# One step of side work per tile, and the second half's convolution inside the first pass, in a two-layer mixture-of-experts kernel

## What is computed

```python
# attention-like convolution: x (2, 3584, 192), 8 heads of 24 channels, 7 taps per token and head
w = softmax(weight_gen)                       # (2, 3584, 8, 7)
out[b, s, h, :] = sum_k w[b, s, h, k] * x_pad[b, s + k, h, :]
# first mixture of experts: 7168 tokens, 8 experts, 192 -> 1024 -> 192, the two best of noisy logits
noisy = x @ w_gate + log1p(exp(x @ w_noise)) * noise
out[t] = sum over the 2 best e of  share_e * (relu(x[t] @ w1[e]) @ w2[e])
# second mixture of experts: the same sizes, the one best expert, times its softmax value
```

## Time and profile before

| | |
|---|---|
| runs | 1349.66, 1350.25, 1351.6 us; median 1350.25 |
| the profiled execution | 1347.76 us, its span 1346.0 us, mean granted clock 0.926 |
| busy: PE, DVE, ACT, POOL | 1165.7, 789.3, 508.5, 507.8 us |
| front, until PE's first expert matmul | 0 to 206.8 us |
| pass 0, pass 1, pass 2, pass 3 | from 206.8, 553.8, 916.8, 1146.8 us |

### The profile page before, as it was taken

The page is one execution under the profiler, slowest core; times in us unless marked ns, Lnnn a source line. Parts: engine busy times, 40 slices in busy tenths (PEclk is TensorE's granted clock), DMA queues, the critical chain, the costliest instruction groups (busy, mean ns, idle before and its releaser), DMA issues.

```text
span 1346.0 us, 25668 instructions
## 1 busy us (share of the span) xinstructions
PE 1165.7 (87%) x8376; PEld 1109.0 (82%) x8377; DVE 789.3 (59%) x1628; ACT 508.5 (38%) x997; POOL 507.8 (38%) x624
## 2 busy tenths in 40 slices
PE   3844799998779999999999988799899859899996
PEld 2531468998779999999999978799899859899996
DVE  9979984655664554544453565554553685455542
ACT  2240125432323444444454233244554324445432
POOL 1000003443334455444433444344433444455543
PEclk9975898998899999999999989899999979999988
DMA  7230133322213333262321243234631383343321
GB/s 221 63 131 4 51 109 100 92 63 75 87 32 95 97 102 99 83 245 83 95 85 53 83 137 107 72 100 150 225 93 61 92 228 91 106 141 106 104 76 31
DMA packets 96257, 136.83 MB, mean 102 GB/s; under 512 B 25930, under 2 KB 75917, under 8 KB 95948
## 3 DMA queue, kind: packets, MB, share of 16 engines
q1 hardware_dynamic: 76652, 92.96, 22.8%
q0 software_dynamic: 19552, 43.30, 10.8%
HBM read 105.00 MB, written 34.54 MB: 104 GB/s over the span
## 4 chain that ended last, share of the span: by engine, by line
PE 67%; DVE 21%; issue 5%; ACT 2%; DMA 2%; DVEq 1%; POOL 1%; SPq 0%; ACTq 0%; POOLq 0%; PEldq 0%
PE ps_y L1211 23%; PE ps_y L1212 10%; DVE prod L525 6%; PE ps_h L1189 6%; PE ps_h L1190 5%; PE ps_h L1193 5%; PE ps_h L1199 5%; PE ps_h L1196 5%; DVE prod L537 3%; PE ps_x L1175 2%; PE ps_x L1176 2%; DVE x_pad L670 2%; DVE x_pad L669 1%; DVE w_hl L737 1%; PE ps_route L1125 1%
## 5 line engine op out<-in xcount | busy, mean ns | idle before, releaser
L1211 PE MATMUL ps_y<-w_hl,h_hi 128*128 128x384 f32 x1480 | 470.5, 380 | 78.2 <-DVE h_lo L752 78.0
L1212 PE MATMUL ps_y<-w_hl,h_lo 128*128 128x192 f32 x1480 | 381.5, 258 | 0.0
L752 DVE SCALAR_TENSOR_TENSOR h_lo<-ps_h,h_hi 128x512 fp32r<-128x512 f32 (+1 forms) x404 | 240.6, 639 | 225.8 <-ACT h_hi L993 217.2
L1211 PEld LDWEIGHTS ps_y<-w_hl,h_hi 128*128 128x128 f32 x1480 | 292.8, 198 | 82.9 <-DVE h_lo L752 82.9
L993 ACT ACTIVATE h_hi<-ps_h 128x512 fp32r<-128x512 f32 (+1 forms) x404 | 204.8, 559 | 310.7 <-PE ps_h L1199 310.7
L1212 PEld LDWEIGHTS ps_y<-w_hl,h_lo 128*128 128x128 f32 x1480 | 297.1, 201 | 0.0
L436 POOL DMA_INDIRECT row<-x_rows,read_now x204 | 209.0, 1025 | 123.2 <-POOL read_now L432 84.2
L1189 PE MATMUL ps_h<-xa_hi,w1a_hi 128*128 128x256 f32 (+1 forms) x808 | 234.4, 290 | 5.1 <-issue 3.7
L1190 PE MATMUL ps_h<-xa_hi,w1a_lo 128*128 128x256 f32 (+1 forms) x808 | 231.4, 286 | 0.0
L1193 PE MATMUL ps_h<-xa_lo,w1a_hi 128*128 128x256 f32 (+1 forms) x808 | 231.0, 286 | 0.0
L1196 PE MATMUL ps_h<-xb_hh,w1b_hl 128*128 128x256 f32 (+1 forms) x808 | 230.7, 285 | 0.0
(11 more groups left out here) (168 smaller groups left out, 1411.2 us busy)
## 6 DMA issues: line engine op xcount, KB each, us to landing
w_raw<-in_moe_w_dram SPq DMA_DIRECT2D x32, 768.0 KB, 6.9
w1a_raw<-in_moe_w_dram SPq DMA_DIRECT2D x32, 512.0 KB
w1b_raw<-in_moe_w_dram SPq DMA_DIRECT2D x64, 256.0 KB, 3.9
x_pad<-in_x_dram SPq DMA_DIRECT2D x2, 2688.0 KB, 10.0
x_rows<-tok SPq DMA_DIRECT2D x14, 384.0 KB, 2.7
x_pad<-y_rows SPq DMA_DIRECT2D x8, 672.0 KB, 11.7
prod<-y_rows SPq DMA_DIRECT2D x8, 672.0 KB, 13.4
x_rows<-tok SPq DMA_DIRECT2D x4, 1344.0 KB, 8.7
```

The source lines that it names most:

```text
L752: nc.vector.scalar_tensor_tensor(out=h_lo[:, i * GF:(i + 1) * GF, 0:rows], in0=ps_h[:, i, :].rearrange("p (f t) -> p f t", f=GF)[:, :, 0:r ...
L1211: nc.tensor.matmul(ps_y[:, u, 0:2 * D], h_hi[:, i, cols], w2_hl[b][:, f, :], start=(i == 0), stop=False)
L1212: last = nc.tensor.matmul(ps_y[:, u, 0:D], h_lo[:, i, cols], w2_hl[b][:, f, 0:D], start=False, stop=(i == FC - 1))
```

## The change

- `convolution(1, ...)` and PE's `front(1, ...)` leave the front. In pass 0, tiles 0 to 13, DVE makes two columns a tile (`conv_column`): one multiply of 1344 elements (7 taps by 192 channels, read from `x_pad` with the tap as the fastest index) and one reduction over the taps. The first half of it (column 0) stands in `side_a`, ahead of the tile's `h_lo`, the second in `side_b`, ahead of the tile's `y`.
- The results of passes 1 and 2's previous half are weighted (ACT) and combined (DVE) four columns a tile. In all three passes ACT copies the tile's columns to a staging place (`stage_columns`), PE transposes them in the next tile (`turn_columns`, after the first 10 of the tile's hidden matmuls), ACT reads them (`read_turned`, between the second and third `h_hi`), and PE makes their logits in the tile after (`score_columns`). The transposes share PSUM with those of the next rows, which therefore wait for a new semaphore `ps_x_free`.
- `place` is cut in three, and the marks are made 14 to a tile (`mark_some`: 7 in `side_a`, 7 in `side_b`), with `find_some` on PE a tile later.
- `load_y` and the stores of `x_rows` (but for half 0's first) move from SP to ACT: `load_y` in tile 0 of passes 1 and 2, the stores at the end of tile 15 of pass 0, in tile 15 of pass 1 and in tile 14 of pass 2.
- ACT and DVE always handle 256 rows, also in a half-full tile; PE still does 128 there. In pass 2 the last tile no longer transposes rows for pass 3: pass 3 begins with it.
- The first expert's weights are split on DVE ahead of `place(0)` (two parts) and behind `list_rows(0)` (the third) instead of within `convolution(1, ...)`.

The table and the main functions:

```diff
+        AHEAD = 4
...
+        COLS = (2, AHEAD, AHEAD)
+        FIRST = (0, 3, 2)
+        LAST = tuple(FIRST[p] + TP // COLS[p] - 1 for p in range(PASSES - 1))
+        SCORE = tuple(LAST[p] + 2 for p in range(PASSES - 1))
+        COUNT = (SCORE[0] + 3, SCORE[1] + 1, SCORE[2] + 1)
+        MARK = (COUNT[0] + 2, COUNT[1] + 3, COUNT[2] + 3)
+        MARKS = 7
+        MARK_STEPS = tuple(TP * choices_of // (2 * MARKS) for choices_of in (2, 1, 1))
+        LIST = tuple(MARK[p] + MARK_STEPS[p] for p in range(PASSES - 1))
...
+            def conv_column(j, i):
+                dve.wait_ge(x_loaded, 96)
+                t = first_column(0, j, 0) + i
+                made = prod[:, i * K * D:(i + 1) * K * D].rearrange("p (d k) -> p d k", k=K)
+                nc.vector.tensor_tensor(
+                    made.rearrange("p (h g) k -> p h g k", g=G),
+                    x_pad[:, bass.ds(t * D, K * D)].rearrange("p (k h g) -> p h g k", h=H, g=G),
+                    taps[1][:, bass.ds(t * H, H), :].unsqueeze(2).broadcast_to([P, H, G, K]),
+                    ALU.mult).then_inc(columns_made, 1)
+                dve.wait_ge(columns_made, j * 2 + (i + 1))
+                nc.vector.tensor_reduce(tok[1][:, bass.ds(t, 1), :].rearrange("p o d -> p (o d)"), made, AX, ALU.add)\
+                    .then_inc(columns_done[1], 1)
...
+            def load_y(p, g0):
+                c = p - 1
+                act.wait_ge(y_scattered, (g0 + 1) * SUBS16)
+                act.wait_ge(found_ready, p + 1)
+                for g in range(GROUPS):
+                    for k in range(2):
...
+                        nc.scalar.dma_start(results[k][:, g * TG:(g + 1) * TG, :], src[:, g * TG:(g + 1) * TG, :])\
+                            .then_inc(y_loaded[c], 16)
+            def weight(p, j):
...
+                act.wait_ge(y_loaded[c], 2 * GROUPS * 16)
...
@@ ACT, tile
                 for i in range(NG):
...
+                    if i == NG // 2 - 1:
+                        side_mid(p, g0, j)
+                        act.sem_inc(ps_x_free, 1)
+                        if ahead is not None:
+                            split_w1a(*ahead)
...
+                side_end(p, j)
@@ DVE, tile
+                side_a(p, j)
                 for i in range(NG):
...
                 if ahead is not None:
                     split_w1b(*ahead)
+                side_b(p, j)
                 dve.wait_ge(y_scattered, (g0 + j + 1) * SUBS16)
@@ DVE, front
+            split_w1a(0, 0)
+            split_w1b(0, 0)
+            for part in range(3):
+                place(0, part)
             for k in range(2):
                 mark_rows(0, k)
             list_rows(0)
-            convolution(1, range(NB))
+            split_w2(0, 0)
             split_rows(0)
@@ ACT, front
-            front(1, range(NB))
             split_rows(0)
@@ PE, tile
                     if place_of(f0) % GF == GF - 1:
                         last.then_inc(h_ps, 2)
+                    if f0 == 0:
+                        side(p, j)
...
                     if i == FC // 4:
-                        transpose_rows(g0 + j + 1)
+                        if p == 2:
+                            with pe.If(j + 1 < n):
+                                pe.wait_ge(ps_x_free, g0 + j + 1)
+                                transpose_rows(g0 + j + 1)
+                        else:
+                            pe.wait_ge(ps_x_free, g0 + j + 1)
+                            transpose_rows(g0 + j + 1)
```

More of the change, by code:

```diff
@@ L748, in tile, with mark_at @@
+            def mark_at(p, j, half):
+                with dve.If(j >= MARK[p]):
+                    with dve.If(j < LIST[p]):
+                        mark_some(p, j, half)
+            def tile(p, g0, n, j, ahead):
+                side_a(p, j)
                 for i in range(NG):
@@ L839, in experts @@
+                    with dve.Fori(b0 + 1, b1) as j:
+                        tile(p, g0, n, j, None)
             def experts(p):
                 g0 = first_tile(dve, p)
+                n = tile_bounds(dve, p, E - 1)[1]
                 last = p + 1 == PASSES
+                if last:
+                    split_rows(g0)
                 with dve.Fori(0, E // 2 - last) as i:
@@ new lines, in weight @@
+            def weight(p, j):
+                c = p - 1
+                act.wait_ge(shared, c + 1)
+                act.wait_ge(y_loaded[c], 2 * GROUPS * 16)
+                t0 = first_column(p, j, -1)
+                for i in range(AHEAD):
+                    t = bass.ds(t0 + i, 1)
+                    column = results[0][:, t, :].rearrange("p o d -> p (o d)")
+                    last = act.activation(column, column, ACT.Copy, scale=share[c][:, 0, t])
+                last.then_inc(weighted[c], 1)
@@ L989, in tile @@
+            def tile(p, g0, n, j, ahead):
                 for i in range(NG):
[L990 to L991 removed]
                     act.wait_ge(h_ps, (g0 + j) * NG + (i + 1))
[L993 removed]
+                    act.activation(h_hi[:, i * GF:(i + 1) * GF, :], ps_h[:, i, :].rearrange("p (f t) -> p f t", f=GF),
@@ L1047, in experts, with section @@
+                act.activation(y_lo[:, :, :], ps_y[:, :, D:2 * D], ACT.Copy).then_inc(y_lo_ready, 1)
+                side_end(p, j)
+            def section(p, g0, n, bounds, s, b, ahead):
+                b0, b1, _ = bounds
+                tile(p, g0, n, b0, (s + 1, 1 - b) if ahead else None)
+                with act.If(b0 + 1 < b1):
+                    with act.Fori(b0 + 1, b1) as j:
+                        tile(p, g0, n, j, None)
             def experts(p):
                 g0 = first_tile(act, p)
+                n = tile_bounds(act, p, E - 1)[1]
@@ L1259, in _ @@
+                if p == 2:
+                    with pe.If(n < STEPS):
+                        with pe.Fori(n, STEPS) as j:
+                            side(p, j)
+            for p in range(PASSES - 1):
+                pe.sem_inc(turned[p + 1], FIRST[p] + 1)
             front(0, range(NB + 1))
@@ L1261, in _ @@
             find_rows(0)
-            front(1, range(NB + 1))
             transpose_rows(0)
```

522 lines of the change are left out of this document (286 added, 236 removed).

## The result

The changed kernel takes 1367.36 us (median; 1366.67 to 1369.26 in 4 runs), the kernel before 1350.01 (1349.66 to 1351.60) beside it. The ratio is 1.0128, with the interval 1.0111 to 1.0146: slower by 17 us, where 48 us less were forecast. The profiled execution took 1367.36, and its span is 1365.6 us.

The account below looks back on a forecast made before the run. PE bounds the passes, DVE's half-1 convolution the stretch before them. Front -64, pass 0 +25, pass 1 -22, pass 2 -5, pass 2 to 3 +4, code +14: -48 from 1347.8, so 1299.8 profiled, 1302 median; range 1268 to 1352.

Parts of the forecast that it names:

- front: Ahead of pass 0: with half 1's convolution and PE's work after it gone, pass 0 starts near 143 us, 64 us less.
- pass 0, excess, with the 14 for code: Pass 0 beyond 9.8 us per full, 7.2 per half tile: 67 to 69 against 44, plus 14 for DVE's code stops.
- tiles 0 to 13: Pass 0's column steps: DVE sets the pace at 11.6 us a full tile; 43 us lost, before code.
- the other tiles: Rest of pass 0: marks plus one section's splits 7 us; `place`, choices and list mostly in DVE's idle time, 5.
- pass 1, excess: Pass 1 beyond its tiles at 9.8 and 7.2 us: 40 against 62, so 22 us less.
- pass 2, excess: Pass 2 beyond its tiles at 9.8 and 7.2 us: 59 against 64, so 5 us less.
- the price of the multiply: DVE's column step in pass 0: 1.5 us for 1344 elements read 768 bytes apart, lower end of 1.5 to 6.3.
- rival A: Pass 0's strided multiply runs at half rate, 3.0 us instead of 1.5, 28 times: +42, 1344 us; chance 0.17.
- Rival B: DVE's longer program stops for instruction fetches at jumps: 45 us instead of 14, 1333 us; chance 0.10.
- The store at tile 15: End of pass 0's tile 15: ACT issues two whole-half stores, 7 us, within the 12 us by which tile 16 suffers.
- The load of the results: `load_y` on ACT in tile 0 of passes 1 and 2: third `h_hi` late, 5.5 us plus 1.5 of clock, 7.
- Rival C: Slower than before: a pass 0 column needs over 4.8 us; multiply 4.5, column 6.1, +84, 1386 us; chance 0.08.

Follow-up runs that it names:

- one copy: The changed kernel with one copy of DVE's tile code per section instead of two, the weight splits under a condition: 1358.45 us, ratio 1.0054.
- the mended kernel: The changed kernel with an unstrided multiply and three contiguous additions, stores of `x_rows` on SP, and one copy of DVE's tile code per section: 1332.45 us, ratio 0.9874.
- the additions alone: The changed kernel with an unstrided multiply and three contiguous additions in place of the strided reduction over taps: 1345.77 us, ratio 0.9980.
- the kernel without the move: The mended kernel with half 1's convolution back ahead of pass 0, so no column step in pass 0: 1347.79 us, ratio 0.9992.
- the kernel with 38: The mended kernel (57 instruction packets) with a tile's marks as a hardware loop instead of repeated code (38 packets): 1374.63 us, ratio 1.0188.

## Why the prediction was wrong

By its own terms, on the profiled executions (1367.4 against the forecast 1299.8, so 68 us are to be found):

| term | forecast | measured |
|---|---|---|
| front | pass 0 starts at 143 | 144.4 |
| pass 0, excess, with the 14 for code | 83 | 117.3 |
| of it tiles 0 to 13 (with the code) | 57 | 67.3 |
| of it tile 16 | 12 | 14.4 |
| of it the other tiles | 14 | 35.6 |
| pass 1, excess | 40 | 63.1 |
| pass 2, excess | 59 | 67.8 |
| pass 2 to 3 (pass 3 against before) | +4 | +4.0 |

(The forecast's 14 for the other tiles of pass 0 is 7 + 5 and the 2 between its 67 and 69.)

**The front was right as a sum, and partly by luck.** 62.4 us against 64. Its landing was mis-sized: the last gather is issued by 136.5 us and PE waits for it until 142.4, so 5.9 us against the 2 assumed. Against that, the list was done no later than before, so that the 1.2 us of the two splits did not come, and the gathers were issued 1.4 us earlier than the sum had it (136.5 against 137.9). The joint of passes 2 and 3 came out at its 4 us.

**The step that failed first is the price of the multiply.** "I take the lower end", 1.5 us, "as most of so short an instruction is overhead": it is 2.56. The row that spoke for more, the scan at 4.7 ns an element (7.4 by the mean of one, 206 ns), was explained away, and the range kept rival A at 0.17. At 28 columns that is 29 us of DVE time, on the engine that sets the pace, and 28 us of pass 0. Rival A had the mechanism and nearly the price (+1.5 a column; it is +1.0). The Trainium skill, Advanced Engine Details and Errata (SBUF Cachelines), says that an access whose neighbours lie in other lines of SBUF pays; the runs agree and give the price, 1.0 us for 1344 elements, in a read of the multiply, a read of the reduction, and a write. Tiles 0 to 13 came out at 67 us and not at 83 only because the forecast's other parts of them were too dear: without the stride they cost 40.9 us in that kernel's trace, code stops included, where 57 were forecast. That is luck: two errors, of 26 and 16 us, in part cancel. The wait was another one than forecast as well. The forecast had PE stand for `h_lo`; it stood for the transposes of the staged columns. And it had the clock near 1.00; the granted clock was 0.88 over these tiles, 0.95 without the stride, and 0.99 with the convolution in front.

**Code.** 14 us were charged, all to pass 0, "since pass 0's loop before shows no such stops". (It has one, of 1.55 us at 452.15.) The experiments bound it: 22 us for code alone in the kernel before, 9 us back for one copy. The stops also fell where the forecast said that slack would hide them: in tile 24 of pass 0 (2.76 and 1.54 us above), in tile 77 of pass 2 (3.39 and 1.83 us, at 1090.2 and 1097.1), and in pass 1, whose excess fell by 9.3 us with one copy. Rival B's mechanism is real, at half of its price or less.

**ACT as a queue.** The store at tile 15 was forecast at 7 us and took 6.6 in the issue; the single term was right. It was short in pass 1, where four issues stand in a row. In its chain:

```profile
747.14 0.39 ACTq L297
747.56 1.47 ACTq L298
749.07 4.16 ACTq L297
753.26 3.01 ACTq L298
```

9.0 us against 6.5; the four of pass 2 took 12.0 against 9. Not all of it is felt: of 28 us of issue, moving the stores alone gave 13 back. The load of the results was forecast at 7 us and cost 6.7 (16.5 in tile 32), but by another wait: PE stands 4.6 us there not for `h_hi` but for the transposes of the next rows, which the new `ps_x_free` holds until ACT's issues are over.

**"Mostly fit into DVE's idle 5.9 us: 5".** Of the net misses this and pass 1 are the largest, 22 and 23 us: the other tiles of pass 0 cost 36 us where 14 were forecast. In tile 17 (17.01 us above) DVE is busy only 9.65 us, yet PE waits 4.3, because the end of `choose_first` and all of `choose_second` stand beside the weight splits and ahead of `h_lo`. DVE's timeline around the seam of tiles 16 and 17:

```profile
390.72 0.39 DVE L574 TENSOR_TENSOR lane<-narrow,iota_e 128x224 f32<-128x224 f32 x1
392.78 0.56 DVE L878 TENSOR_TENSOR y<-ps_y,y_lo 128x384 f32<-128x384 f32 x1 [1.67 <-issue]
393.26 1.75 DVE L782 TENSOR_TENSOR w_hl<-w_raw,w_hl 128x1536 fp32r<-128x1536 f32 x1
...
397.46 0.39 DVE L607 TENSOR_TENSOR lane<-lane 128x224 f32<-128x224 f32 x1
399.07 2.48 DVE L865 SCALAR_TENSOR_TENSOR h_lo<-ps_h,h_hi 128x512 fp32r<-128x512 f32 x4 [1.22 <-issue]
```

The first `h_lo` of tile 17 comes 8.5 us after the tile's start; 2.9 of these are idle of DVE that nothing shown releases (1.67 and 1.22 above). Slack of the whole tile is no slack at the point where `h_lo` is due. That reading is of the trace; a kernel with those steps in another tile was not tried.

**Pass 1 and pass 2.** Of the 23 us by which pass 1 missed, 15.6 are gone in the mended kernel, and 5.2 and 9.3 with the stores and the second copy alone. (With the additions alone, which do not touch pass 1, it is 4.7 shorter, so each of these is good to some 5 us.) In pass 2 the mended kernel's excess is 66.5, the same as after. Its chain names two parts: the stops in tile 77 (2.59 and 1.74 us there, 3.39 and 1.83 after), and the stores, which on ACT are felt in tile 78 and on SP hold back the next expert's weights and are felt in tile 79. How much of the 9 us over the forecast each has stays open.

**Not foreseen:** the 25 us of PE's wait for staged columns. In tiles 0 to 13 it is 23.5 us, 13.3 without the stride, and none where the columns are made in front. So it goes with the column step, as the place where a late column reaches PE. What the staging costs by itself was not tested apart.

**The point estimate and the sign.** Rival C, the one on the slow side, asked for a column over 4.8 us; at 4.1 us, 4.4 with DVE's idle before its two instructions, the kernel was slower all the same, because the terms of pass 0, pass 1 and pass 2 all missed in the same direction. The range let them add only as far as 1352.

## What to carry to other kernels

Side work that is moved under an engine "with slack" has to be priced at the access pattern that it gets there. In this kernel a stride cost about the same in a read, a write and a reduction, and contiguous passes were cheaper though they took more instructions. Then count slack up to the instruction that the bottleneck waits for, not over the tile. And ask what the move does to the program itself: its size in jumps and fetches, and whose queue its DMAs stand in. There was work behind them on SP too. Once these three were mended, the kernel was 1.3% faster than the one before, and by the kernel without the move that gain is the move's.

## What the hardware showed that was not expected

- DVE, 1344 fp32 elements in 128 partitions: 1.55 us contiguous; 2.56 read 768 bytes apart, 2.68 written 28 bytes apart, 2.51 in a reduction that reads 768 bytes apart.
- 115 DVE instructions per copy that never run: 22 us (1.6%) for a kernel whose instruction packets rose from 36 to 104. Yet fewer packets are no measure of time: the kernel with 38 was 42 us slower than the one with 57.
- A hardware loop on DVE around the two instructions of a mark takes 0.79 us a turn, 0.42 more than the same in straight code.
- One store's issue held ACT for 6.01 us. On SP the same store took 9.49 and is not in the chain; but in pass 2 the stores on SP (1.40, 4.23 and 2.65 us, from 1099.5 on, in the kernel with the stores on SP) stood ahead of the weight loads, and the chain runs through them.
